# The first head's queries over two DMA queues, their second copies on GpSimd, and two filler products inside the first hash

## The reference

```python
q_bits = (np.einsum('bhsd,dk->bhsk', q, proj) > 0)
k_bits = (np.einsum('bhsd,dk->bhsk', k, proj) > 0)
mask = q_bucket[:, :, :, None] == k_bucket[:, :, None, :]
scores = np.where(mask, scale * q @ k.T, -1e9)
attn = softmax(scores); out = attn @ v
```

## Time and profile before

| | us |
|---|---|
| median of the runs | 410.65 |
| the profiled execution | 414.38 |
| its span (first to last instruction) | 412.6 |
| PE busy | 399.7 (97%) |
| DVE busy | 250.4 (61%) |
| ACT busy | 202.1 (49%) |
| GpSimd (POOL) busy | 80.7 (20%) |

### The profile page before, as it was taken

How to read it: one execution, slowest core, us unless ns; L and a number is a source line. 1 busy time by engine, 2 the same in 40 slices (tenths; PEclk the granted TensorE clock), 3 DMA queues, 4 the chain that set the end, 5 groups by cost and what they waited for, 6 DMA issues and landing times.

```text
span 412.6 us, 7248 instructions
## 1 busy us (share of the span) xinstructions
PE 399.7 (97%) x2667; PEld 366.6 (89%) x2668; DVE 250.4 (61%) x441; ACT 202.1 (49%) x389; POOL 80.7 (20%) x81
## 2 busy tenths in 40 slices
PE   7999999999999999999999999999999999999995
PEld 3578998998999879899999999999988999899984
DVE  3698889899899561311011111118899998877761
ACT  5778977977788520301101111117667555553541
POOL 0640320330510032274742700000000000000005
PEclk9799999999999999999999999999999999999999
DMA  8492941891700044999899999800000000000003
GB/s 297 169 217 72 264 100 40 268 228 44 252 3 0 2 155 143 414 400 367 309 390 373 346 375 390 313 2 0 2 0 2 1 1 2 0 2 0 0 2 153
DMA packets 15595, 62.85 MB, mean 152 GB/s; under 512 B 2896, under 2 KB 3536, under 8 KB 11344
## 3 DMA queue, kind: packets, MB, share of 16 engines
q1 hardware_dynamic: 14176, 58.51, 41.6%
q0 software_dynamic: 960, 3.15, 2.0%
q10 hardware_dynamic: 432, 0.83, 0.6%
HBM read 49.89 MB, written 3.15 MB: 129 GB/s over the span
## 4 chain that ended last, share of the span: by engine, by line
PE 69%; DVE 13%; ACT 7%; DMA 5%; issue 2%; POOL 2%; POOLq 0%; ACTq 0%; SPq 0%; DVEq 0%
PE ps L727 13%; PE ps L830 12%; PE ps L745 12%; PE ps L805 12%; PE ps L659 5%; PE ps L632 5%; PE ps L545 4%; DVE ptl L1192 3%; DVE nmax L1135 3%; PE ps L615 2%; DMA xg<-rows 2%; ACT prob L915 2%; PE ps L508 2%; ACT pth L953 1%; DMA qq<-in_first 1%
## 5 line engine op out<-in xcount | busy, mean ns | idle before, releaser
L727 PE MATMUL ps<-xs,ring 128*128 x512 | 60.0, 277 | 0.1
L727 PEld LDWEIGHTS ps<-xs,ring 128*128 128x128 f32 x512 | 58.7, 192 | 0.8 <-issue 0.5
L745 PE MATMUL ps<-hs,ring 128*128 128x128 f32 (+1 forms) x512 | 59.2, 276 | 0.0
L745 PEld LDWEIGHTS ps<-hs,ring 128*128 128x128 f32 x512 | 58.5, 192 | 0.0
L1192 DVE TENSOR_TENSOR ptl<-ps,pth 128x384 fp32r<-128x384 f32 x96 | 48.8, 550 | 4.5 <-ACT pth L953 4.4
L953 ACT ACTIVATE pth<-ps 128x384 fp32r<-128x384 f32 x96 | 42.2, 495 | 18.3 <-PE ps L659 17.6
L1135 DVE TENSOR_REDUCE nmax<-ps 128x1 f32<-128x768 f32 x48 | 45.8, 955 | 6.6 <-PE ps L545 5.6
L545 PE MATMUL ps<-ops 128*128 128x384 f32 x192 | 45.8, 361 | 0.8 <-ACT prob L915 0.8
L915 ACT ACTIVATE prob<-ps,nmax 128x768 f32<-128x768 f32 x48 | 43.5, 907 | 3.9 <-DVE nmax L1135 3.9
L805 PE MATMUL ps<-yh,wih 128*128 128x384 f32 x128 | 43.0, 336 | 0.3 <-ACT hc L1036 0.3
L659 PE MATMUL ps<-cfs,prob 128*128 128x128 f32 x288 | 41.5, 277 | 1.9 <-DVE ptl L1192 1.6
(11 more groups left out here) (161 smaller groups left out, 655.7 us busy)
## 6 DMA issues: line engine op xcount, KB each, us to landing
ring<-in_w SPq DMA_DIRECT2D x32, 1024.0 KB, 6.9
winraw<-in_w_in SPq DMA_DIRECT2D x8, 512.0 KB, 6.3
woutraw<-in_w_out SPq DMA_DIRECT2D x8, 512.0 KB
ops<-kh SPq DMA_DIRECT2D x12, 192.0 KB, 3.8
ops<-qh SPq DMA_DIRECT2D x6, 384.0 KB, 6.4
xg<-rows SPq DMA_DIRECT2D x1, 1539.0 KB, 6.9
raw<-in_vt SPq DMA_DIRECT2D x4, 384.0 KB, 5.6
raw<-in_qt SPq DMA_DIRECT2D x3, 384.0 KB, 6.8
```

Source lines behind the costliest of these rows:

```text
L727: last = mm(ps[:, fc // 2, (fc % 2) * WIDE:(fc % 2) * WIDE + W], wa[:, 2 * fc // KF, kd, P * (fc % (KF // 2)):P * (fc % (KF // 2)) + P], x ...
L745: last = mm(ps[:, 4 + half * KD // 2 + k, 0:W], wb[:, half, fc, P * k:P * k + P], hs[:, fc, 0:W], start=(fc == 0), stop=(fc == KF - 1))
```

## The change

SP loads partitions 96 to 127 of qq of head 0, second in its queue; ACT loads partitions 0 to 95, and both count on q0, for which ACT now waits with 32. The copies of q into QA leave ACT and are made by GpSimd with a multiplication by the scale, ahead of its other work: two halves for head 0 after q0, one piece for head 1 after q1, each counting on ch as before. In the hash of head 0, PE runs two fillers into bank 0 between the key's products and the query's.

```diff
--- before.py
+++ after.py
@@ -228,6 +228,7 @@
 
 
         DMASA, DMASB = 10 * 16, 4 * 16
+        EDGE = 96
         PA, PD = 2, 4
         TURN = 4
 
@@ -320,6 +321,7 @@
                 sp.dma_start(raw[:, g % 2, 2, :, :], vt[g, :, :, :]).then_inc(s[f"rv{g % 2}"], 16)
 
             load_head(0)
+            sp.dma_start(early["qq"][EDGE:P, 0, :], first[0, 1, EDGE:P, :]).then_inc(s["q0"], 16)
             sp.dma_start(cbs[:, 0:heads_to], cb[:, 0:heads_to]).then_inc(s["c"], 16)
             sp.dma_start(cfs[:, 0:late_at], cf[:, 0:late_at]).then_inc(s["c0"], 16)
             load_head(1)
@@ -429,6 +431,16 @@
                 hold(gp, s["passed_gp"], s["ka"], 2 * g)
                 nc.gpsimd.tensor_tensor(ql, rk[1], qh, sub).then_inc(s["kl"], 1)
 
+            def q_copy(p, cs):
+
+                nc.gpsimd.tensor_scalar(ops[0:D, p, QA, cs], early["qq"][0:D, p, cs], SCALE, None,
+                                        ALU.mult).then_inc(s["ch"], 1)
+
+            hold(gp, s["passed_gp"], s["q0"], 32)
+            for c in range(2):
+                q_copy(0, slice(c * HALF, c * HALF + HALF))
+            hold(gp, s["passed_gp"], s["q1"], 16)
+            q_copy(1, slice(0, T))
             hold(gp, s["passed_gp"], s["ca"], 5)
             nc.gpsimd.tensor_tensor(ops[0:D, 1, KB, :], early["kk"][0:D, 1, :], ops[0:D, 1, KA, :],
                                     sub).then_inc(s["cp"], 1)
@@ -524,6 +536,8 @@
                     pe.wait_ge(s["cp" if p else "cq"], (c + 1, 1)[p])
                     mm(sums[c], ehi[0:D, 0:HROWS], o[0:D, KB, part[c]], start=False, stop=False,
                        skip_group_check=True)
+                if p == 0:
+                    keep_clock(2, 0)
                 for c in range(2):
                     pe.wait_ge(s["cq"], (c + 3, 5)[p])
                     pe.wait_ge(s["ch"], (c + 1, 3)[p])
@@ -852,8 +866,8 @@
             av = nc.scalar.activation
 
             act.dma_start(eproj[:, :], proj1).then_inc(s["pj"], 16)
-            for p in range(2):
-                act.dma_start(early["qq"][:, p, :], first[p, 1, :, :]).then_inc(s[f"q{p}"], 16)
+            act.dma_start(early["qq"][0:EDGE, 0, :], first[0, 1, 0:EDGE, :]).then_inc(s["q0"], 16)
+            act.dma_start(early["qq"][:, 1, :], first[1, 1, :, :]).then_inc(s["q1"], 16)
             act.preload_act_table_set("natural_log_exp_and_others")
             act.wait_ge(s["pj"], 16)
             av(ehi[:, :], eproj[:, :], ACT.Copy).then_inc(s["pja"], 1)
@@ -866,7 +880,6 @@
             def q_high(p, cs):
 
                 av(ops[:, p, QB, cs], early["qq"][:, p, cs], ACT.Copy, scale=SCALE).then_inc(s["ca"], 1)
-                av(ops[0:D, p, QA, cs], early["qq"][0:D, p, cs], ACT.Copy, scale=SCALE).then_inc(s["ch"], 1)
 
             def head_one(p, c, bank):
 
@@ -878,7 +891,7 @@
             act.wait_ge(s["k0"], 16)
             for c in range(2):
                 k_high(0, both[c])
-            act.wait_ge(s["q0"], 16)
+            act.wait_ge(s["q0"], 32)
             for c in range(2):
                 q_high(0, both[c])
             act.wait_ge(s["k1"], 16)
```

## The result

| | before | after |
|---|---|---|
| median of 12 runs each, us | 410.67 (410.34 to 411.28) | 411.71 (411.35 to 412.16) |
| ratio | | 1.0023 [1.0012, 1.0034] |
| the profiled execution, us | 414.38 | 411.37 |
| its span | 412.6 | 409.6 |

The account below looks back on a forecast made before the run. PE was taken to bound the kernel, busy 97% of the span, with the edits before the first row maximum. Terms -0.1 - 0.4 + 0.35 + 0 - 2.6 = -2.75 took 410.65 to 407.9 us, range 407.2 to 411.1.

Parts of the forecast that it names:

- I take the difference off the median: Base of the sum: changes read from the 414.38 us profiled execution, subtracted from the runs' median of 410.65.
- Step (5): From hash end to first row maximum: fillers keep the clock at 1.00, -2.6 us (bounds 0 and -2.9).
- No clock to gain: Rival: fillers don't carry the clock, or ordinary runs have no late DMA engine and no fall; 410.5 us, chance 0.29.
- (1): Transfer of head 0's qq split over two queues: -0.1 us, near 0; SP's later issues covered, else up to 0.45.
- (2): ACT's second copies removed: head 0's half-copy no longer stands between the QB copies, -0.4 us; head 1's, 0.
- (3): GpSimd's copies, 0.5 us per half, hold DVE's q_low back: +0.35 us (bounds 0 and +2.6).
- (4): Two fillers in the hash: 0 under PE's 0.87 us wait for q_low, +0.46 us if bare.
- (6): After the first row maximum: q_low of head 1 against GpSimd's L421; 0 if DVE gets in first.
- The collision with L421: Rival: GpSimd's L421 goes first and q_low of head 1 waits; gain only -1.0, 409.6 us, chance 0.13.
- The slower rival: GpSimd's copy for head 1 holds DVE out of half 1: hash +0.8, 411.5 us; chance 0.12 without clock gain.
- the profiled time drops and the runs' doesn't: Sign, for the whole kernel, that the prediction is wrong; the other was the clock row still falling near 9.2.

Follow-up runs that it names:

- e1: The kernel before, unchanged, profiled again: 410.76 us, ratio 1.0002.
- f1: The kernel before with head 1's queries loaded first, so that head 0's come late: 415.88 us, ratio 1.0126.
- e6: The changed kernel without its two fillers (split load and GpSimd's copies on the kernel before): 413.00 us, ratio 1.0053.
- f2: The kernel before with head 1's queries loaded first, plus the two fillers in the first hash: 415.22 us, ratio 1.0100.
- e2: The kernel before plus only the two fillers in the first hash: 411.21 us, ratio 1.0006.
- e5: The changed kernel with the copies into QA back on ACT (split load and fillers on the kernel before): 410.71 us, ratio 1.0001.
- e7: The kernel before with GpSimd making the copies into QA as plain copies, without the scale: 410.58 us, ratio 0.9997.
- e8: The kernel before with head 0's two copies into QA made by DVE, ahead of q_low: 410.54 us, ratio 0.9997.
- f4: The kernel before plus the two fillers, with GpSimd making QA's high part as a plain copy from QB: 411.21 us, ratio 1.0010.
- e4: The kernel before plus only GpSimd's copies into QA with the multiplication: 411.41 us, ratio 1.0028.

## Why the prediction was wrong

**What failed first is the base of the sum**, the sentence "I take the difference off the median". 3.7 us lay between the profiled execution and the median. Step (5) wanted 2.6 of just those back, and they aren't in an ordinary run: e1 holds 1.00 without any filler. The size in (5) was right: with a kept clock the row maximum follows the hash end by 2.90 in after (I had 2.86), and f1 prices a lost clock at 2.6. But e1 has 2.89 without a filler, so this is no sign that the fillers give it back. Whether they would have kept the clock in an execution like the old profile stays open: in e6 against after they do, in f2, with later queries, they don't. (The row from which I expected it, 2.21 of 3.00 us busy, was not "no denser" than 2.51 of 3.50 but a little denser, 0.74 to 0.72.) At best it was a true answer about an execution of which there are 3 in a hundred. An execution with no clock to lose I had listed as a rival, "No clock to gain", with the right reason and 0.29, and wrote "Against: no row"; a gap larger than the claimed gain should have made it the likeliest. My 411.6 for the profiled execution, against 411.37, was met by luck: the old profile had lost the clock and the new one hadn't.

**Step by step**, against e1:
- (1) The split, -0.1 (0 at worst): +0.5 in the landing. The bound was wrong too: the step counted what leaves ACT's queue, and not that SP's share queues behind kk and that q0 waits for the later of the two. The late landing that I explained by a single DMA engine's tail was the rare execution's: 6.52 against 5.26 in e1.
- (2) The copies off ACT, -0.4: from landing to the end of both low parts 1.65 (7.44) against 1.97 (7.23), so -0.3. Right, and worth nothing, as PE now waits for something later.
- (3) GpSimd's copies, +0.35 (0.5 us each): 1.17 and 1.25 us each, 2.12 for head 1. This is the term of the sum that was mis-sized. I took "one tensor in" as the mark and leaned on the CAST row; even the two-input row's half, 0.91, which I called the upper end, is too low. It also named the wrong victim: DVE isn't held out, PE waits for the copies themselves. From landing to the start of half 1's product it is 2.83 (8.62 - 5.79) in place of 2.02 (7.28 - 5.26): +0.8.
- (4) The fillers, 0: right in e2's trace (+0.05) and in after's, where PE still waits for GpSimd; bare in e5's, 0.54, where I had a price of 0.46. The runs of e2 (+0.46, interval over zero) leave open which is the usual case.
- (6) The collision with L421 didn't decide anything. DVE's q_low of head 1 got in before it in both kernels, and was itself held by the CAST before it: 1.45 in after and 1.30 in e1, in place of 0.95. Neither is on the chain.

Sum against e1: 0.5 + 0.8 = 1.3, which is the span's difference and the row maximum's; (2) is within the 0.8. The runs show 1.04. The slower rival had the time (411.5) and not the mechanism: the multiplications didn't hold DVE out.

**Which lines would have told it.** My last sentence named the outcome, "the profiled time drops and the runs' doesn't", and the table of times before had both numbers, 410.65 and 414.38.

## What to carry to other kernels

Before a gain is read out of a profiled execution, its own time is put against the median of the runs: what lies between them is a gain that the runs don't have, and here it was larger than the whole forecast. An instruction moved to another engine is priced by a row of the same form on that engine, or its bounds stay wide on the dear side; one input or two is not the form. And two transfers that count on one semaphore land with the later, so a share put behind another load on a second queue can make the whole tile late; whether the queue or the place in it did that here, no run separates.

## What the runs showed of the hardware

- GpSimd's multiplication of a 64x384 float32 tile by a constant into float32r takes 1.17 to 1.25 us, of 64x768 2.12 to 2.14; the plain copy of 64x768 0.82 (e7); DVE does the 64x384 product in 0.35 (e8), ACT the 64x384 copy with a scale in 0.51. Doubling the columns adds 0.9 to the product.
- DVE with two SBUF inputs against GpSimd's CAST or TENSOR_TENSOR: the one that starts second waits for the other. In f4 GpSimd's subtraction is first and keeps its 1.82; DVE's low part, 0.95 alone, starts 1.03 before its end and takes 1.84:

```profile
12.70 1.82 POOL L438 TENSOR_TENSOR ops<-kk,ops 64x768 fp32r<-64x768 f32 x1
```
```profile
13.49 1.84 DVE L1111 SCALAR_TENSOR_TENSOR ops<-qq,ops 64x768 fp32r<-64x768 f32 x1
```

  In e1 each engine is second once. DVE starts 0.48 before the end of a CAST and takes 0.35 more than alone; GpSimd's L421 starts 0.64 before DVE's end and takes 0.51 more:

```profile
12.74 1.30 DVE L1105 SCALAR_TENSOR_TENSOR ops<-qq,ops 64x768 fp32r<-64x768 f32 x1
```
```profile
12.40 0.82 POOL L419 CAST vs<-raw 128x768 fp32r<-128x768 f32 x1
13.40 2.33 POOL L421 TENSOR_TENSOR vs<-raw,vs 128x768 fp32r<-128x768 f32 x1 [0.18 <-POOL vs L419]
```

  Each time the second is longer by the overlap less 0.13 or 0.14 us. The Trainium skill, page SBUF — State Buffer, section Who interferes with whom, has the pair as taken for a whole instruction by the first, the other blocked; these rows agree. GpSimd's multiplication by a constant is another matter: in after DVE's low parts lie wholly beside it (6.37 to 7.44, GpSimd from 6.06 to 8.47) and take 0.60 and 0.55, in e4 0.67 and 0.55, against 0.56. For that form the rule as the page has it, for any GpSimd instruction that reads SBUF, isn't borne out. That is why the port decided nothing for head 0 here.
- Whether the clock is kept over a thin stretch varies between runs of one program (7 of 12 in e6, 3 of 12 in e4, 3 of 94 before), and one profiled execution doesn't show how often: the profiles of e4 and e6 both read 1.00 from 5.5 to 16 us.
